# Three-stage kernel on Trainium2: the order of the start, w3 and wo first, and the PSUM slots of w3 exchanged

## What is computed

```python
q_assign = np.argmax(np.einsum('bhsd,hcd->bhsc', q_n, c_n), axis=-1)   # k_assign likewise
mask = q_assign[:, :, :, None] == k_assign[:, :, None, :]
scores = np.where(mask, scale * np.matmul(q, k.transpose(0, 1, 3, 2)), -1e9)
x = softmax(scores) @ v                        # then 1536 x 512
x = (((x @ w1) * (x @ w2)) @ w3) @ w_out       # w3 1024x1024, w_out (wo) 1024x512
h = x @ w_in
out = (np.maximum(h, 0) + alpha * np.minimum(h, 0)) @ w_out2
```

## Time and profile before

| | us |
|---|---|
| median of three runs | 809.65 (808.96 to 810.26) |
| the profiled execution | 811.73 |
| its span in the trace | 809.9 |
| PE busy | 768.8 (95% of the span) |
| DVE, ACT, POOL busy | 428.4, 336.4, 188.6 |
| mean granted PE clock | 0.983 of full |

### The profile page before, as it was taken

The page is one execution under the profiler, slowest core; times in us unless marked ns, Lnnn a source line. Parts: engine busy times, 40 slices in busy tenths (PEclk is TensorE's granted clock), DMA queues, the critical chain, the costliest instruction groups (busy, mean ns, idle before and its releaser), DMA issues.

```text
span 809.9 us, 12352 instructions
## 1 busy us (share of the span) xinstructions
PE 768.8 (95%) x4290; PEld 719.6 (89%) x4290; DVE 428.4 (53%) x704; ACT 336.4 (42%) x679; POOL 188.6 (23%) x210
## 2 busy tenths in 40 slices
PE   5999998898998998699999999999999999999998
PEld 4878998798988987699999999999999999999997
DVE  5224996797887988353212214357444443443442
ACT  5224977787787888342212114343112112112111
POOL 2220476766776774500000000000000000000000
PEclk9999998999999999989999999999999999999999
DMA  8734463544645322320000001333001001001001
GB/s 282 155 115 99 106 138 83 138 112 116 142 113 129 93 60 57 97 79 27 1 1 1 0 0 57 99 104 105 1 1 40 0 1 40 0 0 39 1 1 39
DMA packets 63572, 54.07 MB, mean 67 GB/s; under 512 B 31264, under 2 KB 51760, under 8 KB 63536
## 3 DMA queue, kind: packets, MB, share of 16 engines
q1 hardware_dynamic: 63536, 53.59, 25.2%
HBM read 31.50 MB, written 3.19 MB: 43 GB/s over the span
## 4 chain that ended last, share of the span: by engine, by line
PE 78%; DMA 6%; POOL 5%; SPq 4%; DVE 3%; ACT 2%; issue 2%; ACTq 0%; POOLq 0%; DVEq 0%
PE slot L564 57%; PE acc L564 15%; PE slot L627 5%; DMA xo<-xf 3%; DMA inverses<-rec 2%; POOL xf L511 2%; POOL xf L507 2%; PE acc L577 1%; ACT ph L885 1%; SPq L301 1%; DVE pl L1109 1%; SPq L302 1%; PE slot L678 1%; DVE w L1166 1%; SPq L267 1%
## 5 line engine op out<-in xcount | busy, mean ns | idle before, releaser
L564 PE MATMUL slot<-xh,w 128*128 128x384 f32 (+1 forms) x1024 | 276.6, 337 | 0.0
L564 PEld LDWEIGHTS slot<-xh,w 128*128 128x128 f32 x1024 | 187.0, 188 | 2.4
L564 PE MATMUL slot<-xl,w 128*128 (+1 forms) x512 | 172.3, 337 | 0.0
L1003 ACT CAST gh<-gf 128x384 fp32r<-128x384 f32 x64 | 32.9, 514 | 204.2 <-PE acc L564 178.2
L1109 DVE TENSOR_TENSOR pl<-slot,ph 128x384 fp32r<-128x384 f32 x192 | 97.6, 549 | 21.0 <-ACT ph L885 20.7
L1103 DVE TENSOR_REDUCE nm<-slot 128x1 f32<-128x768 f32 x96 | 91.3, 951 | 25.2 <-PE slot L564 24.3
L627 PE MATMUL slot<-ident,pf 128*128 128x128 f32 x576 | 84.7, 282 | 17.3 <-DVE pl L1109 16.9
L564 PEld LDWEIGHTS slot<-xl,w 128*128 128x128 f32 x512 | 96.1, 188 | 2.2
L627 PEld LDWEIGHTS slot<-ident,pf 128*128 128x128 f32 x576 | 69.3, 144 | 29.0 <-DVE pl L1109 25.3
L885 ACT CAST ph<-slot 128x384 fp32r<-128x384 f32 x192 | 83.6, 485 | 24.6 <-PE slot L627 23.7
L877 ACT ACTIVATE pf<-slot,nm 128x768 f32<-128x768 f32 x96 | 87.8, 915 | 9.5 <-DVE nm L1103 9.4
(11 more groups left out here) (121 smaller groups left out, 1116.6 us busy)
## 6 DMA issues: line engine op xcount, KB each, us to landing
stage<-in_moe_w SPq DMA_DIRECT2D x16, 256.0 KB, 3.2
stage<-in_moe_w_in SPq DMA_DIRECT2D x16, 256.0 KB, 2.8
stage<-in_moe_w_out SPq DMA_DIRECT2D x16, 256.0 KB, 3.0
qk<-in_q SPq DMA_DIRECT2D x16, 192.0 KB, 3.7
qk<-in_k SPq DMA_DIRECT2D x16, 192.0 KB, 4.3
vn<-in_v SPq DMA_DIRECT2D x16, 192.0 KB, 3.4
stage<-in_moe_w SPq DMA_DIRECT2D x6, 512.0 KB, 4.8
q<-k SPq DMA_DIRECT2D x16, 192.0 KB, 2.7
```

Of the source, the lines that this page charges most:

```text
L564: return nc.tensor.matmul(o, a, b, start=start, stop=stop)
L1003: copy(gh[j % 2][:, :], gf[j % 2][:, :]).then_inc(gh_done, 1)
```

## The change

The queue issues w3 and wo before q, k, v and alpha, and issues w3 tiles 6 and 7 ahead of the masks. PE turns w3 tile 0, then the centroids (into `acc`), then multiplies the first chunk pair of tile 0, then turns w3 tile 1 and goes on with the product. The transposes of alpha, of w3 tiles 2 and 3, and of q and k of heads 0 and 1 follow, the latter two ahead of product tiles 2 and 3, and `cluster` comes after `turn_w3` of tile 5. Even tiles of w3 use slot 1 and odd ones slot 2. The wait for all eight low parts moves from ahead of score 0 to ahead of score 1; score 0 waits for seven. The loops over f are written out, and within them ACT makes the high part of w3 f + 2 ahead of the copy of tile f. DVE's order follows.

```diff
@@ -354,30 +354,31 @@
             sp.dma_start(cn[:, :], cen.rearrange("h c d -> (h c) d")).then_inc(ld_cen, 16)
-            load_qk(0, 0)
-            load_v(0, 0)
-            load_v(0, 1)
-            load_qk(0, 1)
-            sp.dma_start(al16[:, :], alpha.rearrange("(j p) -> j p", p=P)).then_inc(ld_al, 16)
             load_w3(0, 0)
+            load_wo(0)
             load_w3(1, 1)
-            for i in range(NWO):
+            for i in range(1, NWO):
                 load_wo(i)
...
                 sp.dma_start(early[NWO + f - 2][:, :], w3d[f]).then_inc(ld_early[NWO + f - 2], 16)
+            sp.dma_start(al16[:, :], alpha.rearrange("(j p) -> j p", p=P)).then_inc(ld_al, 16)
+            load_qk(0, 0)
+            load_qk(0, 1)
+            for parity in range(2):
+                sp.wait_ge(w3_turned, parity + 1)
+                load_w3(4 + parity, parity)
+            load_v(0, 0)
+            load_v(0, 1)
             for j in range(2):
...
                 next_qk(0, j + 2)
-            for parity in range(2):
-                sp.wait_ge(w3_turned, parity + 1)
-                load_w3(4 + parity, parity)
             for j in range(2):
                 stack_second(0, j)
-            for j in range(2):
-                masks(0, j)
             for parity in range(2):
...
                 load_w3(6 + parity, parity)
+            for j in range(2):
+                masks(0, j)
             for f in range(2):
...
@@ -600,6 +601,8 @@
                     pe.wait_ge(exp_done, tile(it, c - 1))
+                elif c == 1:
+                    pe.wait_ge(w3_lo, NF)
                 if t == 0:
...
@@ -662,17 +665,14 @@
             def turn_w3(f, parity):
-                s = 2 - parity
-                if isinstance(f, int) and f < 4:
-                    source = stage[parity] if f < 2 else early[NWO + parity]
-                    if f < 2:
-                        pe.wait_ge(ld_stage[parity], 16)
-                    else:
-                        pe.wait_ge(ld_early[NWO + parity], 16)
+                s = 1 + parity
+                if f in (2, 3):
+                    source = early[NWO + parity]
+                    pe.wait_ge(ld_early[NWO + parity], 16)
                 else:
                     source = stage[parity]
-                    pe.wait_ge(ld_stage[parity], 8 * (f - parity))
-                if not isinstance(f, int) or f >= 2:
+                    pe.wait_ge(ld_stage[parity], 16 * (f // 2 + 1) if f < 2 else 16 * (f // 2))
+                if f >= 2:
                     pe.wait_ge(w3_lo, f - 1)
...
@@ -690,38 +690,43 @@
                 pe.wait_ge(w3_lo, f + 1)
-                pe.wait_ge(wc_out, f - 1)
+                if f >= 2:
+                    pe.wait_ge(wc_out, f - 1)
                 product_wc(parity, range(NF))
...
             pe.wait_ge(setup_pool, IDENT)
-            for j in range(2):
-                for half in range(2):
-                    turned(0, j, half, True)
+            turn_w3(0, 0)
             pe.wait_ge(setup_act, 1)
-            nc.tensor.transpose(slot[0][0:D, 0, 0:P], cn[:, :], ident[:, :])
+            nc.tensor.transpose(acc[0:D, 0, 0:P], cn[:, :], ident[:, :])
+            for i in range(NWO):
+                if i == 1:
+                    turn_w3(1, 1)
+                pe.wait_ge(piece_lo, i + 1)
+                if i == 0:
+                    pe.wait_ge(w3_lo, 1)
+                product_wc(0, (2 * i, 2 * i + 1))
+                if i == 1:
+                    pe.wait_ge(w3_lo, 2)
+                    product_wc(1, (0, 1))
+                if i >= 1:
+                    product_wc(1, (2 * i, 2 * i + 1))
             pe.wait_ge(ld_al, 16)
-            nc.tensor.transpose(slot[0][:, 1, 0:NJ], al16[:, :], ident[0:NJ, 0:NJ]).then_inc(cen_turned, 1)
-            turn_w3(0, 0)
-            turn_w3(1, 1)
-            pe.wait_ge(table_done, 2)
-            for i in range(NWO):
-                pe.wait_ge(piece_lo, i + 1)
-                for f in range(2):
-                    if i == 0:
-                        pe.wait_ge(w3_lo, f + 1)
-                    product_wc(f, (2 * i, 2 * i + 1))
+            nc.tensor.transpose(acc[:, 1, 0:NJ], al16[:, :], ident[0:NJ, 0:NJ]).then_inc(cen_turned, 1)
             turn_w3(2, 0)
             turn_w3(3, 1)
-            for half in range(2):
-                cluster(0, 0, half, True)
-            with pe.Fori(2, NF // 2) as i:
-                product_tile(2 * i - 2, 0)
-                turn_w3(2 * i, 0)
-                product_tile(2 * i - 1, 1)
-                turn_w3(2 * i + 1, 1)
+            pe.wait_ge(table_done, 2)
+            for f in range(2, NF - 2):
+                if f < 4:
+                    for half in range(2):
+                        turned(0, f - 2, half, True)
+                product_tile(f, f % 2)
+                turn_w3(f + 2, f % 2)
+                if f == 3:
+                    for half in range(2):
+                        cluster(0, 0, half, True)
             for half in range(2):
                 turned(0, 2, half, True)
-            pe.wait_ge(w3_lo, NF)
+            pe.wait_ge(w3_lo, NF - 1)
             for c in range(LEAD):
...
@@ -852,9 +857,9 @@
                 act.wait_ge(w3_turned, f + 1)
-                if not isinstance(f, int) or f >= 2:
+                if f >= 2:
                     act.wait_ge(wc_full, f - 1)
-                copy(w3h[:, parity, :, :], slot[2 - parity][:, :, :].rearrange("p a (g f) -> p (a g) f", g=4)
+                copy(w3h[:, parity, :, :], slot[1 + parity][:, :, :].rearrange("p a (g f) -> p (a g) f", g=4)
                      ).then_inc(w3_hi, 1)
...
@@ -911,9 +916,6 @@
             act.wait_ge(setup_pool, OPERANDS)
-            for j in range(2):
-                for half in range(2):
-                    operands_hi(0, j, half, True)
             w3_hi_part(0, 0)
...
@@ -922,11 +924,11 @@
                 wc_copy(f, f)
-            with act.Fori(2, NF // 2) as i:
-                wc_copy(2 * i - 2, 0)
-                w3_hi_part(2 * i, 0)
-                wc_copy(2 * i - 1, 1)
-                w3_hi_part(2 * i + 1, 1)
+                for half in range(2):
+                    operands_hi(0, f, half, True)
+            for f in range(2, NF - 2):
+                w3_hi_part(f + 2, f % 2)
+                wc_copy(f, f % 2)
             for half in range(2):
...
@@ -1050,19 +1052,19 @@
                 dve.wait_ge(cen_turned, 1)
-                turned_c = slot[0][0:D, 0, 0:P].rearrange("p (h c) -> p h c", h=H)
+                turned_c = acc[0:D, 0, 0:P].rearrange("p (h c) -> p h c", h=H)
                 ordered(nc.vector.memset(f32(ctab[:, :, :, :]), 0.0))
...
                     ordered(copy(ctab[rows, :, 0, cols], turned_c))
-                copy(al[:, :], slot[0][:, 1, 0:NJ])
+                copy(al[:, :], acc[:, 1, 0:NJ])
                 for rows, cols in halves:
...
                 dve.wait_ge(w3_hi, f + 1)
-                tt_(w3l[:, parity, :, :], slot[2 - parity][:, :, :].rearrange("p a (g f) -> p (a g) f", g=4),
+                tt_(w3l[:, parity, :, :], slot[1 + parity][:, :, :].rearrange("p a (g f) -> p (a g) f", g=4),
                     f32(w3h[:, parity, :, :]), ALU.subtract).then_inc(w3_lo, 1)
...
@@ -1132,27 +1134,25 @@
             dve.wait_ge(setup_pool, OPERANDS)
-            for half in range(2):
-                operands_lo(0, 0, half, True)
-            centroid_table()
-            for half in range(2):
-                operands_lo(0, 1, half, True)
             w3_lo_part(0, 0)
...
             w3_lo_part(1, 1)
-            wo_lo(1)
-            for i in range(2, NWO):
+            for i in range(1, NWO):
                 wo_lo(i)
-            w3_lo_part(2, 0)
-            w3_lo_part(3, 1)
+            centroid_table()
+            for f in range(2):
+                w3_lo_part(2 + f, f)
+                for half in range(2):
+                    operands_lo(0, f, half, True)
+            w3_lo_part(4, 0)
+            w3_lo_part(5, 1)
             for half in range(2):
...
                 picks(0, 0, part)
-            with dve.Fori(2, NF // 2) as i:
-                w3_lo_part(2 * i, 0)
-                w3_lo_part(2 * i + 1, 1)
+            for f in range(6, NF):
+                w3_lo_part(f, f % 2)
             for half in range(2):
...
```

## The result

| | before | changed |
|---|---|---|
| median of five runs, us | 810.14 (808.96 to 811.38) | 816.49 (814.23 to 818.75) |
| ratio | | 1.0068 (95%: 1.0045 to 1.0092) |
| profiled execution, its span | 811.73, 809.9 | 814.23, 812.4 |
| the mark (head 3's transposes) | 61.77 | 67.38 |
| from the mark to the end of the span | 748.1 | 745.0 |

A forecast was written before the change was run, and what follows sets the result against it. PE was taken as the bound, busy 95% of the span. Terms 0.85 - 1.37 + 1.31 + 0.12 + 0.65 + 0.6 + 1.0 gave +3.2 us, from 809.65 to 812.9 us, range 810.3 to 816.0.

The forecast's parts named there:

- Front: Start of PE's work: first six products at 9.8, the other 42 at 17.3, 0.85 us later than the 48 before.
- 42 products: Main burst on PE: starts at half clock, whose 1.7 us loss is the same as before and no term.
- Alpha, twelve transposes, table, low part: PE behind the 42 products: +0.12 alpha, +1.31 transposes, +0.65 table wait, +0.6 wait for w3 tile 2's low part.
- w3 tile 6: Its load stands behind four stack transfers on the DMA queue; lands T + 25.7, costing PE +1.0 us, between 0 and 2.2.
- Exchange: w3 slots: the 1.70 us ahead of score 0 go, but head 3's transposes wait; counted 0, gain at most 1.7.
- Masks: Masks of head 0 ahead of score 0: there at T + 32.4, in time, with 1.9 us more before it counts.
- Written-out loops: Loops over product tiles: 0, since tiles of the loop take 5.46 for 24 products, as in straight code.
- the first one: Rival: the clock stays up through the start's two pauses, -3.4 against the forecast, giving 809.4 us; chance 0.1.
- The second (load in time): Rival at w3 tile 6's load: it is in time, 2.2 us are left, giving 811.8 us; chance 0.17.
- third (masks): Rival ahead of score 0: masks over 3 us later become the bound, mark 2 us behind forecast, 814.9; chance 0.12.
- The fourth: Rival at the exchanged slots: head 3's transposes don't wait, so the exchange gains 1.7 us, giving 811.2; chance 0.06.
- the clock column against the pace: PE's first transposes: granted clock reads 1.00, but 0.25 each against 0.109 later says half speed; the forecast followed the spacing.

The follow-up runs named there:

- its repeat: The kernel before, run once more unaltered: 812.08 us in its one run.
- the kernel with two edits: The kernel before with w3 slots exchanged (all-low-parts wait moved to score 1) and head 2 turned and released ahead of w3 tile 7: 805.13 us, ratio 0.995.
- slots back: The changed kernel with w3 slots as before and the wait for all eight low parts ahead of score 0 again: 813.5 us in its one run.
- head 2 ahead of tile 7: The changed kernel with head 2 turned, and its high and low parts made, ahead of those of w3 tile 7: 810.23 us in its one run.
- loads first: The changed kernel with loads of w3 tiles 6 and 7 issued ahead of the stack transfers of heads 0 and 1: 812.63 us, ratio 1.0038.
- alpha early: The changed kernel with alpha loaded behind w3 tile 1 and turned beside the centroids: 816.15 us in its one run.
- w3 tile 1 first: The changed kernel with both first tiles turned first, alpha early, loads first, head 2 ahead of tile 7, plus w3 tile 1 loaded ahead of wo: 803.17 us, ratio 0.9923.

## Why the prediction was right, and where it was off

The direction, the places and their order were right: a later start of the main burst of products, half clock after it, new waits for the table, for the low part of tile 2 and for the load of tile 6, and an idle that moves from score 0 to head 3. By its own steps:

- *Front:* forecast 17.3 for the 42 products, measured 18.42, **0.85 against 1.97, the first term that was mis-sized.** w3 tile 0 landed 3.39 after issue (3.1 taken), and with 0.14 for the signal to PE and 3.64 for the first series ACT, DVE, DVE (3.5 taken) this put the first products at 10.29 and not 9.8. The six products took 2.93 and not 2.7. The second turn took 1.72, at half pace throughout, and not the 1.3 of a clock that rises at 12.8. The second series took 3.48.
- *42 products:* 11.30, forecast 11.23.
- *Alpha, twelve transposes, table, low part:* product tile 2 began 3.76 after T, the end of the 42 products (29.72), forecast 3.8. The waits of 0.44 and 0.38 are what of 0.65 and 0.6 the trace shows as idle; the rest is in the ends of the transposes ahead of them.
- *Product tile 2 itself:* 5.74 after the wait, where I counted 5.46: 0.28, left out.
- *w3 tile 6:* landed at 56.38, T + 26.7, where I took T + 25.7 out of 24.3 to 26.9: **1.0 against 2.0, the second mis-sized term**, 1.81 of idle and 0.22 of slower transposes. Its issue, 51.68, was at T + 22.0 in place of 21.6, and it landed 4.70 after that in place of 4.1. The stacks' last transfer took 3.7 from its issue at 51.04 and so landed near T + 25.0, where I had its bytes gone at T + 24.2; how much tile 7 took of the rate besides is not shown. With the load ahead of the stacks exactly this went.
- *Exchange:* 0 forecast, 0 measured; the edit that gives it its 2.1 was DVE's order, which the forecast had named as what held head 3.
- *Masks:* ready in time, as forecast. *Written-out loops:* nothing seen.

The sum over these is 1.1 + 1.0 + 0.3 over the forecast, 3.2 + 2.4 = 5.6, the shift of the mark between the two profiled executions.

One step came out by luck in part. The forecast took the loss to half clock to be the same in both kernels, and so no term of the difference. In the two first traces it was: 12.60 - 48 x 0.2275 = 1.7 before, 11.30 - 42 x 0.2275 = 1.7 after. But the same front of the kernel before lost 3.0 in its repeat and 0.25 in the kernel with two edits.

The rivals: the clock did fall, at 18.2 and so at the very end of the pause, and the first one fell with it, but its price for the 42 products was near: in the run whose pause was filled they took 1.5 us less, where it had 1.7. The second (load in time) and third (masks) did not happen. The fourth was answered by the slots set back: they gain nothing alone.

On the clock column against the pace I had followed the pace, and the trace bears that out: the granted clock reads 1.00 in 11 to 14 us while six products take 2.93. The Trainium skill ("TensorE: Matmul & The Clock Gate", "Seeing it yourself") warns that the records of this gate are not always to be trusted, which agrees with that row.

## What to carry to other kernels

In this kernel the start is a chain of landings and of hand-overs between engines, and it paid to let the engine that feeds the others do all its feeding work before the first work that depends on their answer: six products put ahead of one turning cost a whole second round of 3.5 us through ACT and DVE, and turning first won even though PE then waited 2.05 us for the load. A lifted wait is worth nothing until the next wait on the same engine is looked at; the exchange of slots paid 2 us only once the release of head 2 was put ahead of the last low part. And a load that is put behind other transfers on a queue takes on their waits: two 512 KB loads behind four transfers that wait for matmuls cost PE 2 us.

## What was not expected of the hardware

How long PE stays at half clock after a pause is not settled by the length of that pause. The same 42 products took 11.20 to 11.39 after 3.49 us of idle in four traces (both of the changed kernel, slots back, head 2 ahead of tile 7), but 12.55 and 12.63 after the same 3.49 us in two others (loads first, alpha early). In these two the second turn had already run at a faster pace, 1.00 and 1.18 in place of 1.51 to 1.72. They took 9.81 and 9.82 after 0.8, and 12.59 after 0.51 in the variant with w3 tile 1 first. The 48 products of the kernel before took 12.60 after 2.90 us of idle, 13.89 after 2.59, and 11.17 after 1.72 with the same front. That is a spread of up to 2.8 us in a start for code that is all but the same, half of what was to be measured.

One thing sorts these traces, and it is not the length of the pause but how long ahead of the burst the clock falls. In the changed kernel, and in the one with its loads first, the windows of PE read:

```profile
18.00:19.00 1.00, 0.58 (x1) 0.61 0.85 299
```

```profile
16.00:17.00 1.00, 0.00 (x0) 0.88 1.00 184
```

The first fell at 18.2 and the products began at 18.42; full clock was back at 21.6. The second fell at 16.8, the products began only at 17.72, and full clock was back only at 23.6. The other traces fall in with one or the other. In the kernel before, its first trace fell at 16.1 with products from 16.45 and was back at 19.5, while its repeat fell at 16.1 with products from 17.10 and was back at 22.9. Where the fall came at most 0.44 us ahead of the burst, the products lost 1.6 to 1.8 us against full pace; where it came 0.8 to 1.0 ahead of it (the repeat, loads first, alpha early, w3 tile 1 first), they lost 3.0 to 3.1. What places the fall, the runs don't show, and no run tests this reading of nine traces. It is another reason to read single terms between two points of a trace, and not marks or totals alone.
